# Four buffers take other SBUF addresses, and two loads of x move ahead of the parts' transfers in SP's program

## The chip, the cores and the metric

The kernel runs on one NeuronCore of a Trainium2 chip. The metric is the device time of one execution in microseconds; the kernel before takes 1141.52 us (median of 3 runs, 1141.49 to 1141.65). Five engines work in parallel and are tied together by semaphores: PE (matrix products), DVE (vector), ACT (activation functions, copies), POOL (a slower vector engine) and SP, which here only issues DMAs.

## The reference

Two stages follow each other. The first mixes each token's row of x (192 columns, 8 groups of 24) with the six rows before it, with weights from a softmax over 7 taps for each group; rows before the start of a batch are zero. The second is an MLP with a squared ReLU:

```python
w = softmax(weight_gen, axis=-1)                       # (4, 4096, 8, 7)
x_pad = concatenate([zeros(B, 6, D), x], axis=1)       # x: (4, 4096, 192)
y[b, s, h, :] = sum over k of w[b, s, h, k] * x_pad[b, s + k, h, :]
h = y.reshape(16384, 192) @ w_in                       # w_in: (192, 2048)
g = s * maximum(h, 0) ** 2 + b
out = g @ w_out                                        # w_out: (2048, 192)
```

All of it is float32. To keep that accuracy on PE, each operand of a product is split in two float32r parts, a rounded value (`_hi`) and the rest (`_lo`), and three of the four part products are summed.

## The kernel before, in words

Partition p holds 128 consecutive tokens. They are worked off in 32 steps (`STEPS`) of 4 tokens per partition, 512 tokens a step. The steps go over token blocks 2, 3, ..., 31 and then 0 and 1: `AHEAD = 2` puts the first two blocks last, since their first rows need the last rows of the partition before (the edge rows), which are loaded in another way.

A step has these stages:
- SP loads the weights (`w_in`) and ten rows of x for each partition (`x_in`, two buffers by parity). DVE does the softmax and the seven taps (line 678 the products, line 693 the sums), then transposes in 32x32 blocks (line 704) and splits the mixed x into parts (`x_parts`, lines 710 and 712). `bounce` on SP writes the parts to DRAM and reads them back transposed, as `xT1s` and `xT2s` (lines 304, 309, 311).
- PE works in four groups of F (g = 0 to 3). In each it does the first product of the group (line 1048: 36 matmuls, in 18 pairs, one for each half of the rows, weights `w1_hi`, `w1_lo`, `w2_hi`, `w2_lo`, moving operand `xT1s` and `xT2s`) and then the second product of the group before (lines 1086 and 1095: 64 matmuls, in 32 pairs, with `g_hi` and `g_lo` as the weights and `wo` as the moving operand).
- Between the two, ACT takes the ReLU from PSUM (line 468), squares it in place (line 472) and rounds the even pairs into `g_hi` (line 479); DVE rounds the odd pairs (line 758) and subtracts for `g_lo` (line 765). `g_hi` and `g_lo` have two buffers each.
- ACT evacuates the sums of a step, POOL adds them and the bias (lines 424 and 428, `add_sums`), and SP stores the result.

The order on each engine is the order in which the program is written. POOL's `add_sums(i)` also waits until DVE has done two tap products of step i + 3, so DVE's progress sets when POOL starts. On DVE the first tap product of a step waits for `x_loaded`. SP's program is one queue: each wait in it holds what stands behind it. For blocks 0 and 1 the loads have two stages: `load_edge_x` issues 12 small DMAs of edge rows (three for each of the 4 batches, one of them zeros), and `load_rest_of_x` waits until all 12 have landed and then loads the rest.

The buffers are allocated one behind the other in the order of the `sb` calls. In the compiled program `w1_raw` is at byte 16512 of each partition, and 16512 is 128 more than a multiple of 2048. The eight weight buffers take 73728 bytes, 36 times 2048. Behind them stand the small buffers, `x_in`, the softmax and tap buffers and `x_parts`; then `xT1s` at byte 135360 (192 more than a multiple of 2048), `xT2s` at 143552, `g_hi` at 151744, `g_lo` at 168128, and `scratch` at 184512, all 192 more than a multiple of 2048. `scratch` holds `r`, the buffer of ReLU and square.

Of the kernel before, what the change touches and what calls it, by code (L numbers as in the profile page):

```python
# [25 lines left out]
F32R = mybir.dt.float32r  # L26
# [3 lines left out]
P = 128  # L30
STEP = 4
N = STEP * P
GROUP = 4
# [5 lines left out]
def mix_and_mlp(nc, x, weight_gen, moe_w_in, moe_w_out, moe_s, moe_b, out):  # L39
# [34 lines left out]
    with ExitStack() as ctx:  # L74
        def sb(name, shape, dt=F32):
            return ctx.enter_context(nc.sbuf_tensor(name, shape, dt))
# [10 lines left out]
        w2_lo = sb("w2_lo", [P, F // 2], F32R)  # L87
        wo_raw = sb("wo_raw", [P, FT, D])
        wo = sb("wo", [P, FT, 2, D], F32R)
        ones = sb("ones", [P, P])  # L90
        zeros = sb("zeros", [B, PAD * D])
        ident = sb("ident", [P, P])
# [15 lines left out]
        acc = sb("acc", [P, STEP, D])  # L108
        attn_b = sb("attn_b", [P, STEP, D2])
        x_parts = sb("x_parts", [P, 2, BLOCKS, STEP, Q], F32R)  # L110
        xT1s = sb("xT1s", [P, 2, 2, N], F32R)
        xT2s = sb("xT2s", [P, 2, 2, N], F32R)
        xT1 = xT1s[:, 0, :, :]
        xT2 = xT2s[:, 0, :, :]
        x_bounce = nc.dram_tensor("x_bounce", [2 * D, N], F32, kind="Internal")


        g_hi = sb("g_hi", [P, 2, GROUP, N], F32R)
        g_lo = sb("g_lo", [P, 2, GROUP, N], F32R)
        scratch = sb("scratch", [P, 2 * PAIR * N + STEP * (4 * D + P)])  # L120
        first_taps = scratch[:, 0:K * STEP * D].rearrange("p (k t d) -> p k t d", k=K, t=STEP)
        used = 2 * PAIR * N
# [121 lines left out]
        def _(sp):  # L244
# [3 lines left out]
            def load_w(block):  # L248
                sp.dma_start(w_in[:, :, :], w_rows[:, bass.ds(block * wcol, wcol)]).then_inc(w_loaded, FETCH)
# [10 lines left out]
            def load_edge_x(block):  # L260

                missing = PAD - STEP * block
                sp.wait_ge(zeros_ready, 1)
                for q in range(B):
                    a = q * batch_rows
                    for first, n in ((a + 1, batch_rows // 2), (a + 1 + batch_rows // 2, batch_rows // 2 - 1)):
                        sp.dma_start(x_in[first:first + n, block, 0:missing, :],
                                     x_rows[first - 1:first - 1 + n, (TOK - missing) * row:TOK * row]).then_inc(x_edge_loaded[block], FETCH)
                    sp.dma_start(x_in[a:a + 1, block, 0:missing, :].rearrange("p t d -> p (t d)"),
                                 zeros[q:q + 1, 0:missing * row]).then_inc(x_edge_loaded[block], FETCH)  # L270

            def load_rest_of_x(block):
                missing = PAD - STEP * block
                sp.wait_ge(x_edge_loaded[block], 3 * B * FETCH)
                sp.dma_start(x_in[:, block, missing:, :], x_rows[:, 0:STEP * (block + 1) * row]).then_inc(x_loaded[block], FETCH)
# [16 lines left out]
            def store(i, block=None):  # L292
                sp.wait_ge(out_ready, i + 1)
                block = i + AHEAD if block is None else block
                for t in range(STEP):
                    sp.dma_start(quarter_rows[:, :, bass.ds(block * (STEP * row) + t * row, row)],
                                 out_sb[t * Q:(t + 1) * Q, :, :]).then_inc(out_stored, FETCH)

            def bounce(n, parity):


                sp.wait_ge(x_parts_ready, n - BY_PE + 1)
                for q in range(P // Q):
                    sp.dma_start(x_bounce[:, q * P:(q + 1) * P].rearrange("(b j) c -> j b c", j=Q),  # L304
                                 x_parts[q * Q:(q + 1) * Q, :, :, :, :].rearrange("j a f t i -> j (a f) (t i)").bitcast(F32)
                                 ).then_inc(x_bounced, FETCH)
                sp.wait_ge(x_bounced, (P // Q) * FETCH * (n - BY_PE + 1))
                by_part = x_bounce[:, :].rearrange("(a d) c -> d a c", a=2)
                sp.dma_start(xT1s[:, parity, :, :].bitcast(F32), by_part[0:P, :, :]).then_inc(xT1_loaded[parity], FETCH)
                for h in range(2):  # L310
                    sp.dma_start(xT2s[h * D2:(h + 1) * D2, parity, :, :].bitcast(F32), by_part[P:D, :, :]).then_inc(xT2_loaded[parity], FETCH)  # L311
# [28 lines left out]
            def edge_loads(i, block):  # L340
                sp.wait_ge(w_shifted, i + 2)
                load_w(block)
                sp.wait_ge(tap_ready, K * (i + 1))
                load_edge_x(block)
# [10 lines left out]
            with sp.Fori(0, (STEPS - 8) // 2) as j:  # L355
# [4 lines left out]
                bounce(2 * j + 6, 0)  # L360
                store(2 * j + 4)
            edge_loads(STEPS - 4, 0)
            bounce(STEPS - 3, 1)
            load_rest_of_x(0)
            store(STEPS - 5)
            edge_loads(STEPS - 3, 1)
            bounce(STEPS - 2, 0)
            load_rest_of_x(1)
            store(STEPS - 4)
            bounce(STEPS - 1, 1)  # L370
            store(STEPS - 3)
# [803 lines left out]
```

## Time and profile before

| | us |
|---|---|
| median of 3 runs | 1141.52 |
| the profiled execution | 1142.02 |
| its span in the trace | 1140.2 |
| PE busy | 1129.5 (99%) |
| DVE busy | 920.1 (81%) |
| ACT busy | 721.3 (63%) |
| POOL busy | 122.8 (11%) |

The span is the time from the first to the last instruction of the trace; the execution's own time is 1.8 us longer. Busy means that an instruction of the engine is under way. Matmuls are pipelined, and their ends are modelled, so on PE the starts are the better measure. An idle time is shown in brackets in front of the instruction that ended it, with what released it.

### The profile page before, as it was taken

What the parts mean: (1) busy time and instruction counts of PE and PEld (TensorE: products, weight loads), DVE (VectorE), ACT (ScalarE), POOL (GpSimd) and SP (SyncE); (2) the same over time, 40 slices, a digit from 0 to 9 for tenths busy, and PEclk for the clock granted to TensorE, in tenths of its full rate; (3) what the DMA queues carried; (4) which work ended last, traced back from release to release, by engine and by line L of the source; (5) the groups of instructions that cost most, each with busy time, mean ns of one, the idle gap of its engine ahead of it and who ended that gap; (6) DMA issues with size and microseconds to landing.
All of it is one profiled execution on the core that took longest, in us unless ns stands there. A gap on an engine that the chain in (4) does not pass through costs nothing.

```text
span 1140.2 us, 31602 instructions
## 1 busy us (share of the span) xinstructions
PE 1129.5 (99%) x12976; PEld 1115.0 (98%) x12976; DVE 920.1 (81%) x1100; ACT 721.3 (63%) x745; POOL 122.8 (11%) x74
## 2 busy tenths in 40 slices
PE   8999999999999999999999999999999999999998
PEld 6999999999999999999999999999999999999897
DVE  8898887778887788877788877888777888778934
ACT  7777656666666566566656665666666566656663
POOL 1100011110111100111101111001111011110111
PEclk9999999999999999999999999999999999999999
DMA  8512334424334333344243343333442433434121
GB/s 255 93 53 66 87 94 110 117 69 112 80 89 117 88 93 94 81 111 117 67 114 79 90 117 83 98 90 83 113 116 65 117 77 92 103 79 110 35 64 30
DMA packets 98060, 106.76 MB, mean 94 GB/s; under 512 B 7576, under 2 KB 78116, under 8 KB 98032
## 3 DMA queue, kind: packets, MB, share of 16 engines
q1 hardware_dynamic: 95200, 103.90, 34.9%
q0 software_dynamic: 2512, 2.26, 1.3%
q8 instruction: 21, 0.34, 0.1%
q10 hardware_dynamic: 320, 0.20, 0.1%
q14 instruction: 7, 0.06, 0.0%
HBM read 70.62 MB, written 35.39 MB: 93 GB/s over the span
## 4 chain that ended last, share of the span: by engine, by line
PE 93%; DVE 4%; issue 1%; DMA 1%; ACT 0%; SPq 0%; DVEq 0%; ACTq 0%
PE hp L1048 44%; PE op L1086 33%; PE op L1095 15%; DVE acc L693 1%; DVE g_lo L765 1%; DVE g_hi L758 1%; DMA x_in<-in_x 1%; DVE scratch L647 0%; DVE tap L678 0%; DMA x_bounce<-x_parts 0%; DMA w_in<-in_weight_gen 0%; DVE scratch L704 0%; SPq L304 0%; SPq L311 0%; DVE scratch L813 0%
## 5 line engine op out<-in xcount | busy, mean ns | idle before, releaser
L1086 PE MATMUL op<-wo,g_hi 64*128 64x384 f32 x4096 | 600.3, 356 | 2.8 <-DVE g_lo L765 2.7
L1095 PE MATMUL op<-wo,g_lo 64*128 64x192 f32 x4096 | 581.3, 247 | 0.0
L468 ACT ACTIVATE scratch<-hp 128x1024 f32<-128x1024 f32 x254 | 255.5, 1019 | 379.1 <-PE hp L1048 369.2
L1095 PEld LDWEIGHTS op<-wo,g_lo 64*128 64x128 f32 x4096 | 476.6, 188 | 0.4
L1086 PEld LDWEIGHTS op<-wo,g_hi 64*128 64x128 f32 x4096 | 469.4, 184 | 5.1 <-DVE g_lo L765 3.4
L765 DVE TENSOR_TENSOR g_lo<-scratch,g_hi 128x1024 fp32r<-128x1024 f32 x255 | 325.3, 1277 | 178.9 <-ACT g_hi L479 174.7
L1048 PE MATMUL hp<-xT1s,w_hi 64*128 64x512 f32 x2048 | 341.5, 390 | 0.6 <-ACT xT1s L446 0.4
L472 ACT ACTIVATE scratch<-scratch 128x1024 f32<-128x1024 f32 x255 | 270.0, 1059 | 6.0
L1048 PE MATMUL hp<-xT1s,w_lo 64*128 64x512 f32 x1024 | 223.6, 391 | 0.0
L1048 PEld LDWEIGHTS hp<-xT1s,w_hi 64*128 64x128 f32 x2048 | 219.3, 184 | 4.3 <-issue 0.6
L678 DVE TENSOR_TENSOR tap<-x_in,w_soft 128x768 f32<-128x768 f32 x186 | 177.3, 954 | 3.2
L693 DVE TENSOR_TENSOR acc<-acc,tap 128x768 f32<-128x768 f32 x184 | 175.2, 952 | 1.2
L1048 PE MATMUL hp<-xT2s,w_hi 64*128 64x512 f32 x1024 | 170.3, 389 | 0.0
L424 POOL TENSOR_TENSOR scratch<-scratch 128x768 f32<-128x768 f32 x30 | 56.3, 1875 | 967.7 <-DVE tap L678 910.4
L479 ACT ACTIVATE g_hi<-scratch 128x1024 fp32r<-128x1024 f32 x126 | 133.7, 1061 | 10.4
L1048 PEld LDWEIGHTS hp<-xT2s,w_hi 64*128 64x128 f32 x1024 | 117.4, 184 | 2.3 <-ACT xT2s L460 0.3
L1048 PEld LDWEIGHTS hp<-xT1s,w_lo 64*128 64x128 f32 x1024 | 117.8, 185 | 1.8
L1048 PE MATMUL hp<-xT2s,w_lo 64*128 64x512 f32 x512 | 111.8, 391 | 0.0
L758 DVE CAST g_hi<-scratch 128x1024 fp32r<-128x1024 f32 x121 | 86.4, 714 | 2.9 <-PE op L1095 2.0
L1048 PEld LDWEIGHTS hp<-xT2s,w_lo 64*128 64x128 f32 x512 | 58.8, 184 | 1.0
L428 POOL TENSOR_TENSOR scratch<-scratch,bias 128x768 f32<-128x768 f32 x30 | 56.7, 1889 | 4.3
L499 ACT ACTIVATE scratch<-op,s_col 128x1536 f32<-128x1536 f32 x30 | 45.9, 1531 | 1.1 <-PE op L1095 1.0
(83 smaller groups left out, 271.5 us busy)
## 6 DMA issues: line engine op xcount, KB each, us to landing
x_in<-in_x SPq DMA_DIRECT2D x29, 960.0 KB, 4.9
x_bounce<-x_parts SPq DMA_DIRECT2D x116, 192.0 KB, 3.5
xT1s<-x_bounce SPq DMA_DIRECT2D x29, 512.0 KB, 3.8
xT2s<-x_bounce SPq DMA_DIRECT2D x58, 256.0 KB, 4.9
out<-scratch SPq DMA_DIRECT2D x124, 96.0 KB, 1.8
w_in<-in_weight_gen SPq DMA_DIRECT2D x32, 112.0 KB, 2.1
wo_raw<-in_moe_w_out SPq DMA_DIRECT2D x4, 384.0 KB, 6.8
wo_sums<-in_moe_w_out POOLq DMA_DIRECT2D x4, 384.0 KB, 7.0
```

The costliest lines, as they stand in the source:

```text
L424: nc.gpsimd.tensor_tensor(out_sums[:, :, 0:D], out_sums[:, :, 0:D], out_sums[:, :, D:2 * D], ALU.add).then_inc(out_added, 1)
L428: nc.gpsimd.tensor_tensor(out_sb[:, :, :], out_sums[:, :, 0:D], bias[:, :].unsqueeze(1).to_broadcast([P, STEP, D]), ALU.add).then_inc(out_ ...
L468: nc.scalar.activation(r[:, b, :], hp[:, PAIR * b:PAIR * (b + 1), :], ACT.Relu).then_inc(relu_done, 1)
L472: nc.scalar.activation(r[:, q % 2, :], r[:, q % 2, :], ACT.Square).then_inc(square_done, 1)
L479: nc.scalar.activation(g_hi[:, q // 2 % 2, 0:PAIR, :], r[:, 0, :].rearrange("p (f n) -> p f n", f=PAIR), ACT.Copy).then_inc(g_hi_even_read ...
L678: nc.vector.tensor_tensor(product.rearrange("p t (h g) -> p t h g", h=H), x_in[:, parity, k:k + STEP, :].rearrange("p t (h g) -> p t h g", ...
L693: nc.vector.tensor_tensor(acc[:, :, :], acc[:, :, :], tap[:, k % 2, :, :], ALU.add).then_inc(sum_ready, 1)
L758: nc.vector.tensor_copy(g_hi[:, buf, tiles, :], pair).then_inc(g_hi_odd_ready, 1)
L765: nc.vector.tensor_tensor(g_lo[:, buf, tiles, :], pair, g_hi[:, buf, tiles, :].bitcast(F32), ALU.subtract).then_inc(g_lo_ready, 1)
L1048: mm = nc.tensor.matmul(hp[:, j, :], w, xt, start=start, stop=stop)
L1086: nc.tensor.matmul(op[:, t, 0:2 * D], g_hi[rows[h], g % 2, j, t * P:(t + 1) * P], wo[rows[h], k, :, :].rearrange("p a d -> p (a d)"), star ...
L1095: mm = nc.tensor.matmul(op[:, t, 0:D], g_lo[rows[h], g % 2, j, t * P:(t + 1) * P], wo[rows[h], k, 0, :], start=False, stop=(k == FT - 1 an ...
```

## The change

The allocations of `xT1s`, `xT2s`, `g_hi` and `g_lo` move up, right behind `wo`. They take 49152 bytes together, 24 times 2048. In the compiled program they stand at 90240, 98432, 106624 and 123008, each 128 more than a multiple of 2048. What stood between `wo` and them moves up by 49152 bytes, so its distance to a multiple of 2048 stays (`x_in` from 96704 to 145856, `x_parts` from 129216 to 178368), and `scratch` stays at 184512.

In SP's program the two calls of `load_rest_of_x` stand in front of the `bounce` that they stood behind.

```diff
         wo = sb("wo", [P, FT, 2, D], F32R)
+        xT1s = sb("xT1s", [P, 2, 2, N], F32R)
+        xT2s = sb("xT2s", [P, 2, 2, N], F32R)
+        g_hi = sb("g_hi", [P, 2, GROUP, N], F32R)
+        g_lo = sb("g_lo", [P, 2, GROUP, N], F32R)
         ones = sb("ones", [P, P])
...
         x_parts = sb("x_parts", [P, 2, BLOCKS, STEP, Q], F32R)
-        xT1s = sb("xT1s", [P, 2, 2, N], F32R)
-        xT2s = sb("xT2s", [P, 2, 2, N], F32R)
...
-        g_hi = sb("g_hi", [P, 2, GROUP, N], F32R)
-        g_lo = sb("g_lo", [P, 2, GROUP, N], F32R)
         scratch = sb("scratch", [P, 2 * PAIR * N + STEP * (4 * D + P)])
...
             edge_loads(STEPS - 4, 0)
+            load_rest_of_x(0)
             bounce(STEPS - 3, 1)
-            load_rest_of_x(0)
             store(STEPS - 5)
             edge_loads(STEPS - 3, 1)
+            load_rest_of_x(1)
             bounce(STEPS - 2, 0)
-            load_rest_of_x(1)
             store(STEPS - 4)
```

The only engine whose instructions change their order is SP. The first place is behind the edge rows of block 0 (the last two of them are the first two rows here). L275 is the rest of x, L304 to L311 are the transfers of `bounce`, L296 is the store.

```order
 L267 DMA x_in<-in_x 15x1152
 L269 DMA x_in<-zeros 1x16x72
+L275 DMA x_in<-in_x 128x768 [waits x_edge_loaded0]
 L304 DMA x_bounce<-x_parts 32x12x128 [waits x_parts_ready]
 L304 DMA x_bounce<-x_parts 32x12x128 x3
 L309 DMA xT1s<-x_bounce 128x2x512 [waits x_bounced]
 L311 DMA xT2s<-x_bounce 64x2x512 x2
-L275 DMA x_in<-in_x 128x768 [waits x_edge_loaded0]
 L296 DMA out<-scratch 32x4x192 [waits out_ready]
```

The load with its wait passes seven DMAs and their two waits. The second place is behind the edge rows of block 1, where the rest of x is twice as large.

```order
 L269 DMA x_in<-zeros 1x16x24
+L275 DMA x_in<-in_x 128x1536 [waits x_edge_loaded1]
 L304 DMA x_bounce<-x_parts 32x12x128 [waits x_parts_ready]
 L304 DMA x_bounce<-x_parts 32x12x128 x3
 L309 DMA xT1s<-x_bounce 128x2x512 [waits x_bounced]
 L311 DMA xT2s<-x_bounce 64x2x512 x2
-L275 DMA x_in<-in_x 128x1536 [waits x_edge_loaded1]
 L296 DMA out<-scratch 32x4x192 [waits out_ready]
```

Here too the load passes the seven DMAs, and now stands behind the wait for its edge rows alone.

## Rows read from the trace of the kernel before

**Rows 1.** The page's busy times of PE: us, share of the span, instructions.
```profile
PE 1129.5 (99%) x12976; PEld 1115.0 (98%) x12976; DVE 920.1 (81%) x1100; ACT 721.3 (63%) x745; POOL 122.8 (11%) x74
```
**Rows 2.** Chain of waits in order of time: start us, us, what (instructions).
```profile
63.05 4.16 PE hp L1048 x36
...
979.05 4.16 PE hp L1048 x36
...
1013.93 3.48 PE hp L1048 x30
...
1087.17 3.01 PE hp L1048 x25
```
**Rows 3.** Timeline of PE, 1020 to 1084 us: start us, us, instruction [idle before <-releaser].
```profile
1045.78 0.44 PE L1086 MATMUL op<-wo,g_hi 64*128 64x384 f32 x2 [0.95 <-DVE g_lo L765]
...
1064.20 0.44 PE L1086 MATMUL op<-wo,g_hi 64*128 64x384 f32 x2 [0.74 <-DVE g_lo L765]
1082.91 0.44 PE L1086 MATMUL op<-wo,g_hi 64*128 64x384 f32 x2 [0.96 <-DVE g_lo L765]
```
**Rows 4.** Timeline of DVE, 981 to 1064 us.
```profile
981.49 0.95 DVE L678 TENSOR_TENSOR acc<-x_in,w_soft 128x768 f32<-128x768 f32 x1
...
988.24 0.68 DVE L758 CAST g_hi<-scratch 128x1024 fp32r<-128x1024 f32 x1
...
1007.70 1.22 DVE L765 TENSOR_TENSOR g_lo<-scratch,g_hi 128x1024 fp32r<-128x1024 f32 x1
...
1018.64 0.96 DVE L678 TENSOR_TENSOR acc<-x_in,w_soft 128x768 f32<-128x768 f32 x1 [2.19 <-DMA x_in<-in_x]
...
1023.41 2.33 DVE L758 CAST g_hi<-scratch 128x1024 fp32r<-128x1024 f32 x1
...
1044.49 1.22 DVE L765 TENSOR_TENSOR g_lo<-scratch,g_hi 128x1024 fp32r<-128x1024 f32 x1
...
1056.12 0.96 DVE L678 TENSOR_TENSOR acc<-x_in,w_soft 128x768 f32<-128x768 f32 x1 [4.34 <-DMA x_in<-in_x]
...
1061.38 2.77 DVE L765 TENSOR_TENSOR g_lo<-scratch,g_hi 128x1024 fp32r<-128x1024 f32 x1
```
**Rows 5.** Timeline of POOL, 983 to 1061 us.
```profile
985.38 1.86 POOL L428 TENSOR_TENSOR scratch<-scratch,bias 128x768 f32<-128x768 f32 x1
...
1022.55 2.65 POOL L428 TENSOR_TENSOR scratch<-scratch,bias 128x768 f32<-128x768 f32 x1
1058.03 2.76 POOL L424 TENSOR_TENSOR scratch<-scratch 128x768 f32<-128x768 f32 x1 [32.83 <-DVE tap L678]
```
**Rows 6.** Timeline of SP's DMA issues, 995 to 1050 us.
```profile
995.96 0.50 SPq L269 DMA_DIRECT2D x_in<-zeros  x1
1005.96 2.61 SPq L304 DMA_DIRECT2D x_bounce<-x_parts  x4
...
1013.15 0.59 SPq L275 DMA_DIRECT2D x_in<-in_x  x1
1025.22 1.79 SPq L296 DMA_DIRECT2D out<-scratch  x4
...
1033.50 0.50 SPq L269 DMA_DIRECT2D x_in<-zeros  x1
...
1049.90 0.59 SPq L275 DMA_DIRECT2D x_in<-in_x  x1
```
**Rows 7.** DMA issues: KB each, median us from issue to landing.
```profile
x_in<-in_x SPq DMA_DIRECT2D x1, 768.0 KB, 6.1
...
x_in<-in_x SPq DMA_DIRECT2D x4, 72.0 KB, 2.3
```
**Rows 8.** Lines 1086 and 1048 on PE: duration ns min/median/max.
```profile
L1086 PEld LDWEIGHTS op<-wo,g_hi x4096: 182/184/193, 21.6 to 1135.2; 64*128 64x128 f32 x196
L1086 PE MATMUL op<-wo,g_hi x4096: 332/357/443, 21.6 to 1135.3; 64*128 64x384 f32 x196
...
L1048 PEld LDWEIGHTS hp<-xT1s,w_hi x2048: 182/184/188, 12.6 to 1125.4; 64*128 64x128 f32 x187
L1048 PE MATMUL hp<-xT1s,w_hi x2048: 384/388/527, 12.6 to 1125.6; 64*128 64x512 f32 x187
```

## The prediction

> **What bounds the kernel now.** I read the page's busy times first: PE is busy for 99% of the span, DVE for 81% [rows 1]. A busy PE is not yet a PE at its peak, so the next view was the chain of waits in order of time, to see whether PE's work is evenly spaced. It is. The first products of the groups start 8.72 us apart from early on: between 63.05 and 979.05 us lie 916.00 us [rows 2], 105 periods of 8.724. A step of four groups takes 4 x 8.72 = 34.88 us. DVE, ACT, POOL and DMAs come and go in each step beside this and don't shift it, so they don't set the pace in the long middle part.
>
> Near the end the spacing breaks. From 1013.93 to 1087.17 us there are eight periods, which would be 69.76 us, and it takes 73.24 [rows 2]: PE loses 3.48 us. PE's timeline shows where: three idle times of 0.95, 0.74 and 0.96 us, each ended by DVE's line 765, the second half of g_lo [rows 3]. They add up to 2.65 us; the starts show 0.83 us more, since each stop also lets the pipelined matmuls run dry. I take the loss by the starts, 3.48.
>
> Why DVE is late stands in its own timeline [rows 4]. The first tap product starts at 981.49 us without a wait. One step later it would come at 981.49 + 34.88 = 1016.37, but comes at 1018.64, after a wait for the DMA of x. Another step later it would come at 1051.25 and comes at 1056.12, after 4.34 us of waiting for the same kind of DMA. A second delay follows from the first: POOL's additions are released by the second tap product. On time, they mostly fall into DVE's idle stretch behind it, and the cast behind it takes 0.68 us (the one at 988.24, with POOL done at 985.38 + 1.86 = 987.24). Late, they collide: the cast takes 2.33 us while POOL's addition at 1022.55 takes 2.65 in place of 1.86, and at 1061.38 a subtraction takes 2.77 us in place of 1.22 [rows 4, 5]. The lateness lasts: the subtraction of 1007.70 us would be due at 1042.58 in the next step and starts at 1044.49, 1.91 us late; the first idle time of PE ends just when it is done, at 1045.7 [rows 3, 4].
>
> The Trainium skill ("SBUF — State Buffer", Who interferes with whom) says that a cast in the two-port mode and a GpSimd instruction exclude each other for a whole instruction. The trace agrees on the cast: POOL ends at 1025.20, and the cast at 1025.74. By that rule a POOL addition that is released on time costs the cast nothing, the same as the 0.68 us row.
>
> **The change, part one: the rest of x goes first.** Before, the load of block 0 was issued at 1013.15 us, behind a bounce that had waited for DVE's parts until 1005.96. The last of its edge rows was issued at 995.96 + 0.50 = 996.46 [rows 6]. Edge rows land 2.3 us after issue [rows 7], so the load can be issued at about 998.8 us. From issue to the tap product it took 1018.64 - 1013.15 = 5.5 us [rows 4, 6]. It is there at 1004.3, needed at 1016.37: 12 us early. The 2.19 us wait goes, and with it the late POOL.
>
> Then POOL ends on time, at 987.24 + 34.88 = 1022.12 us, and the store that waits for it starts 3.1 us earlier than the 1025.22 of before, if nothing else holds it. The edge rows of block 1, all issued at 1034.00 before, are out at 1030.9, landed at 1033.2. The rest of block 1 takes 6.1 us [rows 6, 7] and is there at 1039.3, needed at 1051.25: 12 us early again. The 4.34 us wait goes too.
>
> What is it moved past? Both loads now hold the bounce behind them while they wait for edge rows. That costs nothing: SP is free again at 998.8 + 0.6 = 999.4 us and the bounce is due at 1005.96; the second time at 1033.8, and the bounce is due at 1040.8. The cover is 6.5 and 7 us. If edge rows landed later than that, the bounce would be late by the rest, and PE's step after it has several more us to spare. The store behind the bounce gains 0.6 us of issue time and waits for POOL anyway. The load of block 1 still in flight at 1039.3 is done before the bounce's transfers begin.
>
> With both waits gone, DVE's last steps repeat the steady pattern, in which PE had no idle time in 100 periods. I take the whole 3.48 us. The bounds: nothing at all below, and 3.5 above, since PE has no more to gain from DVE there. Behind 1087 us all moves up as it is.
>
> **Part two: the addresses.** Four buffers now start 128 bytes behind a multiple of 2048 in place of 192, and lie next to the weights. No row shows the same buffer at two addresses, but the kernel before has operands of both kinds. Weights at 128 (w_hi) load in 182 ns at least and 184 in the median, weights at 192 (g_hi) in 182 and 184: no difference [rows 8]. The moving operand at 192 (xT1s, 512 columns) takes at least 384 ns, the one at 128 (wo, 384 columns) at least 332; that is 52 ns for 128 columns, 0.41 ns each, one column per cycle of 2.4 GHz, with nothing left over for either place [rows 8]. So I take zero. On ACT, DVE and the DMAs a small change would be hidden behind PE.
>
> The price if this is wrong is high, since there are 12976 / 2 = 6488 pairs of matmuls [rows 1]: 1 ns per pair is 6.5 us. From below, the nearest bound is the difference between the two products. 18 pairs of the first take about 4.16 us [rows 2], 231 ns each against 213 for 512 columns at one column per cycle, an excess of 18. The other 32 pairs take 8.72 - 4.16 = 4.56 us, 142.5 ns against 120 in the mean (384 and 192 columns), an excess of 22.5. If the g buffers' place were the reason for the 4.5 ns, 4096 pairs would give back 18 us. From above there is no such row; the spread of the load's median to its longest in normal flow, 184 to 188 ns for w_hi, would be 4 ns per pair and 26 us.
>
> **The rivals.**
>
> A. The forecast: the two x waits go, the addresses do nothing. The span is 1140.2 - 3.5 = 1136.7 us; the profiled execution 1142.02 - 3.5 = 1138.5; from the median, which is 0.5 below the profiled execution, 1141.52 - 3.48 = 1138.0 us.
>
> B. Another late producer takes the place. PE's idle times are ended by DVE, and DVE has its last weights and edge softmax in the same stretch. If the first PE stop (its start late by about 1.3 of the 3.48 us, a share of 0.95 / 2.65) stayed, 1139.3 us; if all stayed, 1141.5. Against it speaks that the steady steps have the same instructions on DVE in the same order and that x is 12 us early by the sum. This rival also covers the case that the reorder does little of what it says.
>
> C. Slower: the matmul and the weight load now read from neighbouring regions (wo 65664 to 90240, g behind it up to 139392), where before g lay over 60000 bytes away. If this costs each of the 4096 pairs of the second product something, the reorder's gain is eaten at 3.48 us / 4096 = 0.85 ns per pair. At 1.5 ns per pair it is 1141.5 + 6.1 - 3.5 = 1144.2 us. For it speaks only that PE has no slack anywhere. Against it: the 8.72 us stay the same whether DVE, ACT and the DMAs write or not, and the weights' load is 184 ns for both kinds of buffer [rows 2, 8].
>
> The Trainium skill ("TensorE: Matmul & The Clock Gate", Step-by-step) says that PE reads weights and the moving operand through two independent read ports. By that rule C would add nothing and the time would be that of A; no row of this trace has the two close together, so it lowers the chance of C without deciding it.
>
> D. Faster by the addresses: the 4.5 ns come from the g buffers' place. Then 18 us go beside the 3.5: 1120 us. A tenth of it would be 1136.2.
>
> **How the numbers follow.** A has 0.74, B 0.11, C 0.08, D 0.07. A change within 0.2% (2.3 us) can't be told from none. A and D are faster: 0.81. B counts as no change: 0.11. C is slower: 0.08. The time is A's, 1138.0 us. Its own range is 1137.3 to 1139.2, for residues of the three stops. The range with two in ten left out reaches up into B, to 1141.2, and down to a small effect of D, 1136.5.
>
> **What would show it.** Right: the tap products behind the x loads of blocks 0 and 1 have no wait for a DMA; PE's three idle times near the end are gone; POOL's last additions that DVE's taps release take 1.85 us each; from 1013.9 us on, eight periods take 69.8; the load of block 0 is issued near 999 us. For the addresses: the period stays at 8.72 us from the start on, and the shortest weight load at 182 ns. Wrong: a period other than 8.72 in the middle of the trace, which would move the time by about 1.3 us for each 0.01 us of it (some 127 groups); or an idle time of PE near 1044, 1062 or 1080 us that some other instruction of DVE ends; or a bounce that starts later than the parts are ready.

## The result, and the profile after

The changed kernel takes 1132.47 us (median of 6 runs) against 1141.51 us of the kernel before (6 runs): 9.0 us less, a ratio of 0.9919 with a 95% interval of 0.9907 to 0.9931. The forecast was 1138.0 us, with a range of 1136.5 to 1141.2. The sign was right; the size was not, and the time lies outside the range. The ratios go by the fast executions alone: one of the six of the changed kernel took 2771.79 us and is left out (the other five lie between 1132.37 and 1132.50, with a median of 1132.46), and so is one of the kernel before, 1793.40 us, in a later group of runs. The profiled execution takes 1132.5 us, its span is 1130.7.

I read the chain of waits first, in order of time. Its columns are those of [rows 2]: start, length, what.

```profile
62.85 4.15 PE hp L1048 x36
71.52 4.15 PE hp L1048 x36
...
982.55 4.15 PE hp L1048 x36
991.23 4.15 PE hp L1048 x36
...
1043.27 4.15 PE hp L1048 x36
1051.94 4.15 PE hp L1048 x36
...
1112.65 4.15 PE hp L1048 x36
```

Two things have changed. Near the end the spacing stays even: from 991.23 to 1112.65 us lie 14 periods (the time from one group's first product to the next) in 121.42 us, 8.673 each, where before eight periods in that stretch took 3.48 us too long [rows 2]. And the period itself is 8.67 us in place of 8.72 all through the trace. The page's busy times show PE as full as before:

```profile
PE 1123.6 (99%) x12976; PEld 1029.0 (91%) x12976; DVE 916.5 (81%) x1100; ACT 721.2 (64%) x745; POOL 120.5 (11%) x74
```

So the gain has two terms: the 3.5 us of the end, as forecast, and 0.047 us on each of the 121 periods between 62.85 and 1112.65 us, 5.7 us, where the forecast had zero. Together they are 9.2 us; the medians differ by 9.0, the spans of the two traces by 9.5.

The end first. SP's issues, then DVE's first tap products for blocks 0 and 1:

```profile
990.84 0.50 SPq L269 DMA_DIRECT2D x_in<-zeros  x1
992.69 0.36 SPq L275 DMA_DIRECT2D x_in<-in_x  x1
1000.82 2.61 SPq L304 DMA_DIRECT2D x_bounce<-x_parts  x4
...
1025.10 0.50 SPq L269 DMA_DIRECT2D x_in<-zeros  x1
1026.77 0.36 SPq L275 DMA_DIRECT2D x_in<-in_x  x1
1035.49 2.61 SPq L304 DMA_DIRECT2D x_bounce<-x_parts  x4
```

```profile
1011.06 0.95 DVE L678 TENSOR_TENSOR acc<-x_in,w_soft 128x768 f32<-128x768 f32 x1
...
1017.80 0.68 DVE L758 CAST g_hi<-scratch 128x1024 fp32r<-128x1024 f32 x1
...
1045.86 0.95 DVE L678 TENSOR_TENSOR acc<-x_in,w_soft 128x768 f32<-128x768 f32 x1
...
1050.96 1.73 DVE L765 TENSOR_TENSOR g_lo<-scratch,g_hi 128x1024 fp32r<-128x1024 f32 x1 [3.28 <-ACT g_hi L479]
1052.62 0.68 DVE L758 CAST g_hi<-scratch 128x1024 fp32r<-128x1024 f32 x1
```

The loads of x now go out at 992.69 and 1026.77 us, eight and nine us ahead of the bounce, and the tap products have no bracket for a DMA any more (before, 2.19 and 4.34 us [rows 4]). The casts behind them take 0.68 us, not 2.33 [rows 4]. POOL is released on time and runs mostly in DVE's idle stretch. The subtraction at 1050.96 still overlaps POOL's second addition and takes 1.73 us, not 1.22; the steady steps of the kernel before have the same (1.67 us at 986.65).

```profile
1012.96 1.84 POOL L424 TENSOR_TENSOR scratch<-scratch 128x768 f32<-128x768 f32 x1 [30.86 <-DVE tap L678]
1014.95 1.85 POOL L428 TENSOR_TENSOR scratch<-scratch,bias 128x768 f32<-128x768 f32 x1
1047.77 1.85 POOL L424 TENSOR_TENSOR scratch<-scratch 128x768 f32<-128x768 f32 x1 [30.97 <-DVE tap L678]
```

Now the period. PE's durations say nothing of it. The weight load of `g_hi` and its matmul, duration min/median/max in ns:

```profile
L1086 PEld LDWEIGHTS op<-wo,g_hi x4096: 182/184/194, 21.5 to 1125.9; 64*128 64x128 f32 x196
L1086 PE MATMUL op<-wo,g_hi x4096: 329/356/442, 21.7 to 1126.0; 64*128 64x384 f32 x196
```

The load's 182/184 is that of before [rows 8], while the groups follow each other in less time. A pipelined instruction's duration is not its price; the distance between starts is.

### The profile page after: what moved, and what is told of

Its sections match the earlier page's. It is cut to its first block, busy times and chain, and to the rows that moved or that the text cites. A ratio compares the mean times of both kernels' runs of the same rounds, so it can differ in the third digit from the quotient of the medians.

```text
span 1130.7 us, 31602 instructions
## 1 busy us (share of the span) xinstructions
PE 1123.6 (99%) x12976; PEld 1029.0 (91%) x12976; DVE 916.5 (81%) x1100; ACT 721.2 (64%) x745; POOL 120.5 (11%) x74
## 4 chain that ended last, share of the span: by engine, by line
PE 98%; DVE 1%; DMA 0%; ACT 0%; issue 0%; DVEq 0%
PE hp L1048 47%; PE op L1086 35%; PE op L1095 16%; DVE scratch L647 1%; DMA w_in<-in_weight_gen 0%; DVE scratch L813 0%; DVE scratch L809 0%; DVE scratch L783 0%; ACT xT1s L446 0%; PE hp L945 0%; PE op L964 0%; PE hp L939 0%; DVE w_soft L638 0%; DVE w_exp L626 0%; ACT w_exp L442 0%
## 5 line engine op out<-in xcount | busy, mean ns | idle before, releaser
L1086 PE MATMUL op<-wo,g_hi 64*128 64x384 f32 x4096 | 590.3, 355 | 0.2
L1095 PE MATMUL op<-wo,g_lo 64*128 64x192 f32 x4096 | 517.6, 247 | 0.0
L1095 PEld LDWEIGHTS op<-wo,g_lo 64*128 64x128 f32 x4096 | 398.0, 188 | 4.6
L1086 PEld LDWEIGHTS op<-wo,g_hi 64*128 64x128 f32 x4096 | 390.6, 184 | 5.5 <-issue 0.3
L1048 PE MATMUL hp<-xT1s,w_hi 64*128 64x512 f32 x2048 | 322.8, 391 | 0.6 <-ACT xT1s L446 0.4
L1048 PEld LDWEIGHTS hp<-xT1s,w_hi 64*128 64x128 f32 x2048 | 185.6, 185 | 29.6 <-issue 0.6
L1048 PE MATMUL hp<-xT1s,w_lo 64*128 64x512 f32 x1024 | 203.2, 389 | 0.0
L479 ACT ACTIVATE g_hi<-scratch 128x1024 fp32r<-128x1024 f32 x126 | 133.6, 1061 | 10.4
L1048 PEld LDWEIGHTS hp<-xT2s,w_hi 64*128 64x128 f32 x1024 | 97.8, 184 | 21.2 <-ACT xT2s L460 0.3
L1048 PEld LDWEIGHTS hp<-xT1s,w_lo 64*128 64x128 f32 x1024 | 98.1, 184 | 19.9
L1048 PE MATMUL hp<-xT2s,w_lo 64*128 64x512 f32 x512 | 101.2, 388 | 0.0
```

Source lines behind the costliest of these rows:

```text
L479: nc.scalar.activation(g_hi[:, q // 2 % 2, 0:PAIR, :], r[:, 0, :].rearrange("p (f n) -> p f n", f=PAIR), ACT.Copy).then_inc(g_hi_even_read ...
L1048: mm = nc.tensor.matmul(hp[:, j, :], w, xt, start=start, stop=stop)
L1086: nc.tensor.matmul(op[:, t, 0:2 * D], g_hi[rows[h], g % 2, j, t * P:(t + 1) * P], wo[rows[h], k, :, :].rearrange("p a d -> p (a d)"), star ...
L1095: mm = nc.tensor.matmul(op[:, t, 0:D], g_lo[rows[h], g % 2, j, t * P:(t + 1) * P], wo[rows[h], k, 0, :], start=False, stop=(k == FT - 1 an ...
```

## The experiments

The runs were made in five groups, each timed together with the kernel before on one chip. Its medians were 1141.68 to 1141.89 us in these groups and 1141.51 in that of the result, so a difference of less than 0.4 us between two groups says nothing. A remainder is the address at which a buffer starts, modulo 2048. "New order" is the changed kernel's order on SP. "The weights" are the buffers with the parts of w1, w2 and `wo`; "the four buffers" are `xT1s`, `xT2s`, `g_hi` and `g_lo`. All diffs are against the changed kernel and are cut; a pad of 16 floats is 64 bytes. Where a pad moves what stands behind it, another one behind the four buffers fills up to a multiple of 2048, so that all other buffers keep their remainders; it is not always shown.

**The order alone.**

```diff
         wo = sb("wo", [P, FT, 2, D], F32R)
-        xT1s = sb("xT1s", [P, 2, 2, N], F32R)
-        xT2s = sb("xT2s", [P, 2, 2, N], F32R)
-        g_hi = sb("g_hi", [P, 2, GROUP, N], F32R)
-        g_lo = sb("g_lo", [P, 2, GROUP, N], F32R)
...
         x_parts = sb("x_parts", [P, 2, BLOCKS, STEP, Q], F32R)
+        xT1s = sb("xT1s", [P, 2, 2, N], F32R)
+        xT2s = sb("xT2s", [P, 2, 2, N], F32R)
...
+        g_hi = sb("g_hi", [P, 2, GROUP, N], F32R)
+        g_lo = sb("g_lo", [P, 2, GROUP, N], F32R)
```

> Only SP's order is changed, the four buffers stay where they were. If the two parts of the change add up (reorder 3.5 us, addresses the rest), 1138.0 us, with a period of 8.72 us between the first products and no idle time of PE near the end. If the addresses are innocent and all of the gain came with the order, 1132.5 us and a period of 8.67 us.

1138.42 us, ratio 0.9971 [0.9959, 0.9982]: 3.3 us less than before. PE waits for nothing behind 900 us, and the period is still the old one:

```profile
202.91 4.16 PE hp L1048 x36
211.63 4.16 PE hp L1048 x36
220.35 4.16 PE hp L1048 x36
```

**The addresses alone.**

```diff
             edge_loads(STEPS - 4, 0)
-            load_rest_of_x(0)
             bounce(STEPS - 3, 1)
+            load_rest_of_x(0)
             store(STEPS - 5)
             edge_loads(STEPS - 3, 1)
-            load_rest_of_x(1)
             bounce(STEPS - 2, 0)
+            load_rest_of_x(1)
```

> Only the four buffers are moved, SP's order is that of before. If the parts add up, about 1136 us (1132.5 + 3.5), with a period of 8.67 us and the three idle times of PE near the end. If the addresses do nothing, 1141.5 us and a period of 8.72 us.

1136.19 us, ratio 0.9951 [0.9934, 0.9968]: 5.5 us less than before. The period is 8.67 us (first fence), and the three idle times of PE are there, from its timeline (second fence):

```profile
201.93 4.15 PE hp L1048 x36
210.60 4.15 PE hp L1048 x36
219.28 4.15 PE hp L1048 x36
```

```profile
1040.36 0.44 PE L1086 MATMUL op<-wo,g_hi 64*128 64x384 f32 x2 [0.96 <-DVE g_lo L765]
1058.65 0.45 PE L1086 MATMUL op<-wo,g_hi 64*128 64x384 f32 x2 [0.65 <-DVE g_lo L765]
1077.38 0.45 PE L1086 MATMUL op<-wo,g_hi 64*128 64x384 f32 x2 [0.96 <-DVE g_lo L765]
```

3.3 and 5.5 add up to 8.8 of the 9.0, which is equal within the differences between groups: the two parts work apart from each other.

**Only x, only g.** The new order, with one pair of buffers behind `wo` (remainder 128) and the other behind `x_parts` (192).

```diff
         wo = sb("wo", [P, FT, 2, D], F32R)
         xT1s = sb("xT1s", [P, 2, 2, N], F32R)
         xT2s = sb("xT2s", [P, 2, 2, N], F32R)
-        g_hi = sb("g_hi", [P, 2, GROUP, N], F32R)
-        g_lo = sb("g_lo", [P, 2, GROUP, N], F32R)
...
         x_parts = sb("x_parts", [P, 2, BLOCKS, STEP, Q], F32R)
+        g_hi = sb("g_hi", [P, 2, GROUP, N], F32R)
+        g_lo = sb("g_lo", [P, 2, GROUP, N], F32R)
```

> SP's new order; only xT1s and xT2s stand behind the weights, at 128 more than a multiple of 2048; g_hi and g_lo stay at their old place (192 more). If PE's pace depends on where g lies as weights of the second product (most of the shorter period is in the second product, 4.57 to 4.53 us), 1138 us or little less (the first product's part, 0.003 us x 127 = 0.4 us). If it depends on xT, 1132.5 us.

1133.45 us, ratio 0.9927 [0.9911, 0.9944]. The expectation had leaned to g (1138 us), and this was wrong: x alone brings 5.0 of the 6.0 us that separate 1138.42 from 1132.47.

```diff
         wo = sb("wo", [P, FT, 2, D], F32R)
-        xT1s = sb("xT1s", [P, 2, 2, N], F32R)
-        xT2s = sb("xT2s", [P, 2, 2, N], F32R)
         g_hi = sb("g_hi", [P, 2, GROUP, N], F32R)
         g_lo = sb("g_lo", [P, 2, GROUP, N], F32R)
...
         x_parts = sb("x_parts", [P, 2, BLOCKS, STEP, Q], F32R)
+        xT1s = sb("xT1s", [P, 2, 2, N], F32R)
+        xT2s = sb("xT2s", [P, 2, 2, N], F32R)
```

> SP's new order; only g_hi and g_lo stand behind the weights, at 128 more than a multiple of 2048; xT1s and xT2s are at 192 more. If g's place sets the pace, 1132.5 to 1133 us and a period of 8.67 to 8.68 us. If xT's place does, 1138 us.

1134.28 us, ratio 0.9934 [0.9918, 0.9951]: g alone brings 4.1 us, and the time fits neither of the two expected. The two chains, x behind `wo` first:

```profile
210.77 4.12 PE hp L1048 x36
219.45 4.12 PE hp L1048 x36
```

```profile
211.13 4.16 PE hp L1048 x36
219.81 4.16 PE hp L1048 x36
```

With x moved the first product takes 4.12 us and the second 8.68 - 4.12 = 4.56, as before. With g moved the first takes 4.16, as before, and the second 8.68 - 4.16 = 4.52 (8.69 in the mean over 45 periods, 4.53). Each product follows its own operand. But the gains don't add up: 5.0 and 4.1 are 9.1 us, and both together bring 6.0. With both at 128 the first product takes 4.15 us, not 4.12. PE's timeline shows where the difference lies. With x alone moved, the pairs of the first product start 227 ns apart from the fourth on; in the changed kernel they do so only from the eleventh on, and the second to the tenth are 231 ns apart in the mean. Why they are slower there is not shown.

**Place or remainder.** Four runs separate the two things that the change had altered at once, the place among the other buffers and the remainder. First the near place with the old remainder, 192:

```diff
         wo = sb("wo", [P, FT, 2, D], F32R)
+        pad_a = sb("pad_a", [P, 16])
...
         g_lo = sb("g_lo", [P, 2, GROUP, N], F32R)
+        pad_b = sb("pad_b", [P, 496])
```

> The order of buffers and of SP as in the changed kernel, but a pad of 64 bytes behind wo puts xT1s, xT2s, g_hi and g_lo at 192 more than a multiple of 2048 (what follows moves by 2048 in all). If the 64 bytes matter, the time goes back to that of the new SP order alone, 1138.4 us. If the neighbourhood (the range of addresses) matters, it stays at 1132.5 us.

1138.45 us, ratio 0.9971 [0.9959, 0.9982]. Then the old place with remainder 128 (the four buffers behind `x_parts`):

```diff
         x_parts = sb("x_parts", [P, 2, BLOCKS, STEP, Q], F32R)
+        pad_c = sb("pad_c", [P, 496])
+        xT1s = sb("xT1s", [P, 2, 2, N], F32R)
+        xT2s = sb("xT2s", [P, 2, 2, N], F32R)
+        g_hi = sb("g_hi", [P, 2, GROUP, N], F32R)
+        g_lo = sb("g_lo", [P, 2, GROUP, N], F32R)
+        pad_d = sb("pad_d", [P, 16])
```

> The old order of buffers with SP's new order, but a pad of 1984 bytes in front of xT1s puts the four buffers at 128 more than a multiple of 2048, far from the weights. If the 64 bytes matter, 1132.5 us. If the neighbourhood matters, 1138.4 us.

1132.42 us, ratio 0.9918 [0.9901, 0.9934]. The neighbourhood does nothing; 64 bytes do all of it. Third, the old place with remainder 0 (`pad_c` of 464 floats, `pad_d` of 48):

```diff
+        pad_c = sb("pad_c", [P, 464])
```

> As the one before, but the four buffers start at multiples of 2048 exactly. If what counts is that a buffer starts at a multiple of 128 (or of a larger power of two), 1132.5 us or less. If what counts is the distance to the weights' remainder of 128, 1138.4 us or another time. If the neighbourhood matters, 1138.4 us.

1146.00 us, ratio 1.0037 [1.0023, 1.0051]: slower than before, in spite of the new order. A round address is the worst so far. Its chain shows both products longer, 4.21 and 4.57 us (first fence), and its weight load the old durations (second fence; line 1088 is the changed kernel's line 1086):

```profile
212.99 4.21 PE hp L1050 x36
221.77 4.21 PE hp L1050 x36
```

```profile
L1088 PEld LDWEIGHTS op<-wo,g_hi x4096: 182/184/194, 21.6 to 1139.3; 64*128 64x128 f32 x196
```

Fourth, the old place with only x at 128 (`pad_c` of 496 floats, and 16 more between `xT2s` and `g_hi`):

```diff
+        pad_c = sb("pad_c", [P, 496])
...
         xT2s = sb("xT2s", [P, 2, 2, N], F32R)
+        pad_e = sb("pad_e", [P, 16])
         g_hi = sb("g_hi", [P, 2, GROUP, N], F32R)
```

> SP's new order and the old places, but only xT1s and xT2s at 128 more than a multiple of 2048, g_hi and g_lo at 192 more. If the 64 bytes matter, it repeats the run with only x behind the weights: 1133.5 us, a first product of 4.12 us and a second of 4.56. If the neighbourhood does, 1138.4 us and 4.16 us.

1133.53 us, ratio 0.9928 [0.9911, 0.9945], as near the weights.

**Alone, or against the weights.** In the next four the buffers stand in the changed kernel's order, with pads. The four buffers and the weights, all at 192:

```diff
+        pad_f = sb("pad_f", [P, 16])
         w1_raw = sb("w1_raw", [P, F])
```

> As the changed kernel, but a pad of 64 bytes in front of all weights: weights, xT1s, xT2s, g_hi and g_lo all at 192 more than a multiple of 2048 (PE's operands have the same remainder again, but another one). If the remainders of the two operands of a matmul must agree, 1132.5 us. If the remainder of x and g alone counts (192 worse than 128), 1138.4 us or another time.

1132.45 us, ratio 0.9918 [0.9900, 0.9936]. The same 192 that cost 6.0 us costs nothing once the weights have it too. Weights at 128 and the four buffers 256 bytes on, at 384:

```diff
         wo = sb("wo", [P, FT, 2, D], F32R)
+        pad_a = sb("pad_a", [P, 64])
```

> Weights at 128 as in the changed kernel, xT1s, xT2s, g_hi and g_lo at 384 more than a multiple of 2048, that is 256 bytes on. If the pattern repeats within 256 bytes (or a fraction of it), 1132.5 us. If it repeats only with a longer step such as 2048, as slow as or slower than 1138.4 us.

1132.40 us, ratio 0.9918 [0.9901, 0.9935]. 256 bytes are as good as none. Now 64 bytes before the weights' remainder:

```diff
         wo = sb("wo", [P, FT, 2, D], F32R)
+        pad_a = sb("pad_a", [P, 496])
```

> Weights at 128, xT1s, xT2s, g_hi and g_lo at 64 more than a multiple of 2048. The distance to the weights is 64 bytes the other way. If only the size of the distance counts, 1138.4 us as at 192. If the time climbs with the amount by which the buffers stand before the weights' remainder (0 gave 1146.0), about 1139 to 1142 us. If it is a matter of being a multiple of 128 or not, 1138.4 us, but then the 1146.0 at 0 stays unexplained.

1143.45 us, ratio 1.0014 [1.0005, 1.0024]: the other direction costs 11.0 us, not 6.0, and none of the expected values came. The chain puts nearly all of it into the first product, 4.23 us; the second, 8.76 - 4.23 = 4.53, is as good as with none:

```profile
212.48 4.23 PE hp L1050 x36
221.24 4.23 PE hp L1050 x36
```

The four buffers and the weights, all at 0:

```diff
+        pad_f = sb("pad_f", [P, 480])
         w1_raw = sb("w1_raw", [P, F])
```

> As the run with all at 192, but all at multiples of 2048 exactly: weights and xT1s, xT2s, g_hi, g_lo. If the operands' remainders must agree, 1132.5 us. If it was the 0 itself that cost time with x and g at 0 and the weights at 128, 1146.0 us.

1132.48 us, ratio 0.9919 [0.9901, 0.9936]. With these two the remainder by itself is out: 0, 128 and 192 are equal when both operands have them.

**Which operands, and how fine.** All the weights shared one remainder in each of these runs. Here `wo` and g are at 192, the first product's weights and xT at 128:

```diff
+        pad_g = sb("pad_g", [P, 16])
         wo = sb("wo", [P, FT, 2, D], F32R)
+        pad_h = sb("pad_h", [P, 496])
         xT1s = sb("xT1s", [P, 2, 2, N], F32R)
         xT2s = sb("xT2s", [P, 2, 2, N], F32R)
+        pad_i = sb("pad_i", [P, 16])
         g_hi = sb("g_hi", [P, 2, GROUP, N], F32R)
         g_lo = sb("g_lo", [P, 2, GROUP, N], F32R)
+        pad_b = sb("pad_b", [P, 496])
```

> w1 and w2 parts and xT1s, xT2s at 128 more than a multiple of 2048; wo and g_hi, g_lo at 192 more. If what must agree are the two operands of the same matmul (w with xT, wo with g), 1132.4 us and a period of 8.67 us. If all that PE reads must agree, or g with the first product's weights, about 1133.5 to 1138.4 us, a second product of 4.56 us.

1130.87 us, ratio 0.9903 [0.9887, 0.9920]. That is 1.6 us under the changed kernel's 1132.47, which was not timed in the same group (the kernel before took 1141.71 us in this one and 1141.51 in the other, so the difference is not the chip's). The period is 8.66 us, the first product 4.13:

```profile
210.44 4.13 PE hp L1052 x36
219.10 4.13 PE hp L1052 x36
```

The period fits: 0.013 us less on some 127 periods is 1.7 us. So it is the two operands of the same product that must agree, and the kernel gains a little more when the second product's two buffers stand 64 bytes further than the first's. Then finer distances from the weights, 32 bytes on (`pad_a` of 8 floats):

```diff
+        pad_a = sb("pad_a", [P, 8])
```

> Weights at 128, xT1s, xT2s, g_hi, g_lo at 160, 32 bytes on. If the distance acts in steps of 64 bytes, 1132.4 us. If it acts evenly, about 1135.4 us, half way to the 1138.4 of 64 bytes.

1146.68 us, ratio 1.0042 [1.0025, 1.0059]. 32 bytes before (`pad_a` of 504 floats):

```diff
+        pad_a = sb("pad_a", [P, 504])
```

> Weights at 128, xT1s, xT2s, g_hi, g_lo at 96, 32 bytes before. If the distance acts in steps of 64 bytes counted from the lower edge, 1143.4 us (as 64 before); if evenly, about 1138 us; if anything within 32 bytes is free, 1132.4 us.

1145.82 us, ratio 1.0035 [1.0023, 1.0048]. 96 bytes on (`pad_a` of 24 floats):

```diff
+        pad_a = sb("pad_a", [P, 24])
```

> Weights at 128, xT1s, xT2s, g_hi, g_lo at 224, 96 bytes on. If it acts in steps of 64 bytes, 1138.4 us; if evenly, between the 1138.4 us of 64 bytes and the 1146.0 of 128, 1142 us.

1146.73 us, ratio 1.0043 [1.0026, 1.0059]. All three missed what I had expected. The cost doesn't grow with the distance and has no steps of 64: it is 14.2, 13.4 and 14.3 us at +32, -32 and +96, more than at either +64 or -64.

Last, the distance between the two products' sets. `wo` and g at 256:

```diff
+        pad_g = sb("pad_g", [P, 32])
         wo = sb("wo", [P, FT, 2, D], F32R)
+        pad_h = sb("pad_h", [P, 480])
         xT1s = sb("xT1s", [P, 2, 2, N], F32R)
         xT2s = sb("xT2s", [P, 2, 2, N], F32R)
+        pad_i = sb("pad_i", [P, 32])
```

> w1, w2 and xT at 128, wo and g at 256 more than a multiple of 2048: operands agree within each product, the two products' sets are 128 bytes apart. If where the sets meet (a load of one product under a matmul of the other) the distance counts as within a product, this is the worst of them, above 1132.5 us. If any distance frees them, 1130.9 us.

1132.68 us, ratio 0.9918 [0.9902, 0.9935]: the same as with one remainder for all, within the differences between groups. And at 64:

```diff
+        pad_g = sb("pad_g", [P, 496])
         wo = sb("wo", [P, FT, 2, D], F32R)
+        pad_h = sb("pad_h", [P, 16])
         xT1s = sb("xT1s", [P, 2, 2, N], F32R)
         xT2s = sb("xT2s", [P, 2, 2, N], F32R)
+        pad_i = sb("pad_i", [P, 496])
```

> w1, w2 and xT at 128, wo and g at 64 more than a multiple of 2048: the sets 64 bytes apart the other way. If only the size of the distance counts, 1130.9 us as at 192; if its sign does, 1132.5 us or more, since within a product -64 cost 11.0 us and +64 cost 6.0.

1133.44 us, ratio 0.9925 [0.9908, 0.9942]. Of the three distances between the sets only +64 beats zero, by 1.6 us; -64 loses 1.0.

The runs in one table, all with SP's new order; the columns are the remainders in bytes. They hold for the start of a buffer. The slices that the matmuls read begin multiples of 512 bytes (w, xT, g) or 768 bytes (`wo`) behind it, by the kernel's index expressions, so modulo 256 they all keep the buffer's distance, and modulo 2048 they don't.

| w1, w2 | xT | wo | g | us |
|---|---|---|---|---|
| 128 | 192 | 128 | 192 | 1138.42, 1138.45 |
| 128 | 128 | 128 | 192 | 1133.45, 1133.53 |
| 128 | 192 | 128 | 128 | 1134.28 |
| 128 | 128 | 128 | 128 | 1132.47, 1132.42 |
| 192 | 192 | 192 | 192 | 1132.45 |
| 0 | 0 | 0 | 0 | 1132.48 |
| 128 | 384 | 128 | 384 | 1132.40 |
| 128 | 64 | 128 | 64 | 1143.45 |
| 128 | 0 | 128 | 0 | 1146.00 |
| 128 | 160 | 128 | 160 | 1146.68 |
| 128 | 96 | 128 | 96 | 1145.82 |
| 128 | 224 | 128 | 224 | 1146.73 |
| 128 | 128 | 192 | 192 | 1130.87 |
| 128 | 128 | 256 | 256 | 1132.68 |
| 128 | 128 | 64 | 64 | 1133.44 |

**What the signs mean.** So far a distance was counted from the weights to the four buffers. But x is the moving operand of the first product, and g the weight operand of the second. So +64 puts the moving operand 64 bytes above the other, modulo 256, in the first product and 64 bytes below it in the second. The next table counts from the operand that is loaded as weights to the moving one, by product. Its times are the distances between the first start of a product and the first start of the next one in PE's timeline, in the mean over the groups between 200 and 960 us, for the runs that moved the four buffers together with the weights at 128.

| moving less loaded, bytes | first product, us | second product, us |
|---|---|---|
| 0 or 256 | 4.15 | 4.53 |
| +64 | 4.16 | 4.53 |
| -64 | 4.23 | 4.56 |
| 128 | 4.21 | 4.57 |
| +32, -32 | 4.22, 4.21 | 4.57, 4.57 |
| +96 | 4.22 | |
| -96 | | 4.56 |

The two products agree: +64 lies within 0.01 us of distance 0, and all else costs 0.06 to 0.08 us in the first product and 0.04 to 0.05 in the second. The 4.15 us hold the slow first pairs; against the 4.12 us of the run with x alone at distance 0, +64 costs the first product 0.04 us. The run at 1138.4 us has its first product at +64 and its second at -64, that at 1143.45 the other way round. The case with both at +64 (xT at 192, g at 64) was not run. Starts are needed here too, since a chain piece can mislead: in the run at 384 the matmuls of a pair start 90 ns apart and the two products overlap, and its chain gives the first product 4.24 us where the starts give 4.15, at the period of the changed kernel.

```profile
201.74 4.24 PE hp L1050 x36
210.41 4.24 PE hp L1050 x36
```

## Why the prediction was wrong, step by step

**The end of the trace: right.** The forecast took 3.48 us for the late loads of x; the order alone measured 3.3 (1141.68 to 1138.42), and its 1138.42 us lie 0.4 above the 1138.0 forecast for that part. In that run each step came as it was written: the loads issued at 997.81 and 1032.04 us (forecast 998.8 and 1033.2), no wait for x at the two tap products, POOL on time, casts of 0.68 us, no idle time of PE, the bounces at 1005.89 and 1040.76 us (due at 1005.96 and 1040.8). Only the landing was off, to the good side: the load of block 1 took 4.1 us where 6.1 had been assumed. It takes 4.0 to 4.3 us in all runs with the new order and 5.9 in the one with the addresses alone, so the order is what shortens it; whether because the bounce is no longer in its way is not shown.

**Rival B (another late producer):** not seen. PE's three idle times behind DVE's line 765 are gone in the run with the order alone and in the changed kernel, and no other has come in their place.

**The addresses: wrong, and this is the step that failed.** "So I take zero" is 5.5 us by the run with the addresses alone, and 6.0 us between the two runs with the new order (1138.42 and 1132.47). That is 0.9 ns for each of the 6400 pairs of the two products; the prediction had priced 1 ns a pair at 6.5 us and given it no weight in the sum. The reasoning had two faults, and the runs show both.
- It compared one operand at a time: weights at 128 against weights at 192, moving operands at 192 against those at 128. What counts is the distance between a product's two operands. In the kernel before it was 64 bytes for both products, in opposite directions, so the trace held each product at one distance only.
- It compared durations. The weight load takes 182 ns at least and 184 in the median in both kernels and also in the run at 1146.00 us (182/184/194), whose period is 0.11 us longer than the changed kernel's. Only the distance between starts shows the pace. The prediction's 0.41 ns a column from the shortest matmuls, "with nothing left over for either place", was such a duration too, while by its own sum each pair took 18 to 22.5 ns longer than its columns. The one view of starts that I used, the period's evenness, shows that nothing disturbs PE from outside; it can't show a cost that is in every period alike.

**Rival C (the neighbourhood costs time):** refuted. Near and far give 1138.45 and 1138.42 us at 192, 1132.42 and 1132.47 at 128. An address could cost time all the same, though by its remainder: the four buffers at 0 with the weights at 128 gave 1146.00.

**Rival D (faster by the addresses):** right in kind, with a chance of 0.07, but sized at 18 us against 5.5 to 6.0. It had ascribed the excess of the second product over the first, 4.5 ns a pair, to g's place. With g matched, the second product goes from 4.56 to 4.53 us, 1 ns a pair; the rest of that excess stays. The first product, which the rival had left out, gains more when x alone is matched, 4.16 to 4.12 us.

The Trainium skill ("TensorE: Matmul & The Clock Gate", Step-by-step) gives PE two independent read ports, one for the weights and one for the moving operand. The prediction had set this against rival C, and the runs agree that the region of the addresses does not matter. They do not agree that the two operands' addresses are without effect on each other: with the region fixed, moving one operand of each product by 32 bytes against the other costs 14.2 us. The measurement decides, though it does not show that the two reads are where the time goes.

The Trainium skill ("SBUF — State Buffer", Who interferes with whom) has a DVE cast in the two-port mode and a GpSimd instruction exclude each other. The casts of 0.68 us with POOL on time, against 2.33 us beside a late POOL, agree with it.

## What to carry to other kernels

Where PE is the bound and its weights and moving operand are both float32r in SBUF, try the same address modulo 256 for the two operands of each product, and then try one product's pair of operands 64 bytes further on than the other's; where the buffers start moved this kernel by up to 1.3% (1132.4 to 1146.7 us). Other kernels and types were not measured. Round addresses are no aim in themselves. And a steady period is no proof of a full-speed period: compare spacing with the columns it should take, and ask of every "no difference" in a trace whether the trace holds the contrast at all.

## What was not expected of the hardware

- PE's pace for pairs of float32r matmuls on two halves of the rows depends on the distance between the two operands' addresses, equal at 0 and 256 bytes (1132.47 and 1132.40 us). The whole spread with all weights at one remainder is 1132.4 to 1146.7 us, 1.3% of the kernel.
- The cost does not grow with the distance. With the four buffers moved together, +64 costs 6.0 us, -64 costs 11.0, 128 costs 13.5, and +32, -32 and +96 cost 13.4 to 14.3. Counted by product, from the loaded operand to the moving one, +64 costs the least (0.01 us or less against distance 0, or 0.04 in the first product against the run with x alone), and every other distance that was run costs more.
- The pace has nothing to do with how far apart the two matmuls of a pair start: they start 3 ns apart in the changed kernel, 50 ns in the run with the addresses alone and 90 ns in that at 384, and the period is 8.673 us in all three. In the kernel before they are 50 ns apart from 200 us up to the first of the three idle times near the end and 3 behind it, and the period is 8.72 us in the long stretch and again behind the last idle time.
- What stays open: which two reads meet. The weights of the next matmul are loaded while the current one streams (in the changed kernel PEld is busy for 91% of the span beside PE's 99%), and that the two streams get in each other's way in the memory is a guess; no run separates the loads from the matmuls. Nor was it tried whether single matmuls over all 128 rows, or other types, behave alike.
